# Clustered attention and two expert layers: where the first head's operands come from, and in which order TensorE takes its first work

## The reference

```python
q_assign = argmax(einsum('bhsd,hcd->bhsc', q_n, c_n), -1)      # q: 2 x 8 heads x 768 x 64, 16 clusters per head
k_assign = argmax(einsum('bhsd,hcd->bhsc', k_n, c_n), -1)      # q_n, k_n, c_n: rows divided by their norms
mask = q_assign[..., :, None] == k_assign[..., None, :]
scores = where(mask, q @ k.T / sqrt(D), -1e9)
attn = softmax(scores) @ v                                     # x: 1536 tokens x 512
x = gate * (relu(x @ w1[e]) @ w2[e])                           # e: the best of 8 experts for each token
out = ((x @ w_a) * (x @ w_b)) @ w_out
```

## Time and profile before

| | us |
|---|---|
| median of 3 runs | 815.81 (815.75 to 816.17) |
| the profiled execution | 815.89 |
| its span, first to last instruction | 814.1 |
| PE busy | 804.4 |
| DVE busy | 455.1 |
| ACT busy | 361.0 |
| POOL busy | 365.8 |

### The profile page before, as it was taken

One profiled execution on the slowest core, in us unless ns is written; L12 is line 12 of the kernel. 1 busy time (PEld: TensorE's weight loads), 2 busy tenths in 40 slices (PEclk: granted clock), 3 DMA queues, 4 the chain that ended last, 5 costly groups with the idle time before them and its releaser, 6 DMA issues.

```text
span 814.1 us, 13192 instructions
## 1 busy us (share of the span) xinstructions
PE 804.4 (99%) x4414; PEld 677.7 (83%) x4415; DVE 455.1 (56%) x721; ACT 361.0 (44%) x742; POOL 365.8 (45%) x308
## 2 busy tenths in 40 slices
PE   8999999999999999999999999999999999999997
PEld 5899999999997688888888888888888888888886
DVE  6987987987997989998866004531212112121211
ACT  6877877877886344334343443111212111121112
POOL 6788988988982355455455634000311002010001
PEclk9999999999999999999999999999999999999999
DMA  6563363363243577788667304300101000010001
GB/s 182 135 184 95 102 185 93 101 185 94 63 120 92 169 236 241 245 253 249 200 205 233 95 35 108 113 0 14 38 3 53 1 14 13 1 52 0 1 1 52
DMA packets 48665, 86.62 MB, mean 106 GB/s; under 512 B 17856, under 2 KB 19904, under 8 KB 48624
## 3 DMA queue, kind: packets, MB, share of 16 engines
q1 hardware_dynamic: 41888, 69.36, 29.5%
q0 software_dynamic: 3856, 11.33, 4.8%
q10 hardware_dynamic: 2880, 5.39, 1.7%
HBM read 73.29 MB, written 11.30 MB: 104 GB/s over the span
## 4 chain that ended last, share of the span: by engine, by line
PE 79%; issue 16%; DMA 2%; POOL 1%; DVE 1%; SPq 0%; POOLq 0%; ACT 0%; DVEq 0%; ACTq 0%
PE bank L1679 9%; PE bank L1749 9%; PE bank L1492 8%; PE bank L1646 7%; PE bank L1648 7%; PE bank L1647 7%; PE bank L1686 4%; PE bank L1461 4%; PE bank L1753 4%; PE bank L1482 4%; PE bank L1508 4%; PE bank L1510 3%; PE bank L1520 2%; PE bank L1419 2%; PE bank L1693 2%
## 5 line engine op out<-in xcount | busy, mean ns | idle before, releaser
L1383 DVE TENSOR_TENSOR ab_raw<-bank,a_sb 128x512 f32<-128x512 f32 x35 | 24.2, 691 | 187.7 <-PE bank L1648 187.7
L410 DVE CAST w_split<-stage 128x1024 fp32r<-128x1024 f32 x68 | 68.5, 1007 | 72.9 <-PE bank L1686 53.9
L1133 DVE TENSOR_REDUCE neg_max<-bank 128x1 f32<-128x768 f32 x96 | 91.2, 951 | 28.7 <-PE bank L1482 28.2
L414 DVE TENSOR_TENSOR w_split<-stage,w_split 128x1024 fp32r<-128x1024 f32 x72 | 98.3, 1369 | 2.4
L1101 DVE TENSOR_TENSOR pT_lo<-bank,pT_hi 128x384 fp32r<-128x384 f32 x192 | 97.3, 547 | 2.7 <-ACT pT_hi L847 2.6
L847 ACT ACTIVATE pT_hi<-bank 128x384 fp32r<-128x384 f32 x192 | 84.2, 491 | 32.0 <-PE bank L1492 30.2
L867 ACT ACTIVATE probs<-bank,neg_max 128x768 f32<-128x768 f32 x96 | 87.0, 907 | 11.6 <-DVE neg_max L1133 11.6
L714 POOL TENSOR_TENSOR hT_lo<-hT_raw,hT_hi 128x512 fp32r<-128x512 f32 x38 | 54.9, 1446 | 79.1 <-ACT hT_raw L926 78.9
L1492 PE MATMUL bank<-ident,probs 128*128 128x128 f32 x576 | 79.8, 274 | 0.9 <-DVE pT_lo L1101 0.9
L986 ACT ACTIVATE a_sb<-bank 128x512 f32<-128x512 f32 x35 | 20.9, 597 | 134.9 <-PE bank L1648 134.9
L1749 PE MATMUL bank<-w_split,hT_hi 128*128 (+1 forms) x304 | 79.5, 403 | 0.0
(11 more groups left out here) (264 smaller groups left out, 1736.7 us busy)
## 6 DMA issues: line engine op xcount, KB each, us to landing
stage<-w SPq DMA_DIRECT2D x64, 512.0 KB, 4.5
q_raw<-qT SPq DMA_DIRECT2D x32, 192.0 KB, 3.7
k_raw<-kT SPq DMA_DIRECT2D x32, 192.0 KB, 3.9
sorted_y<-y_sb ACTq DMA_DIRECT2D x19, 257.0 KB, 5.0
q_pair<-qT SPq DMA_DIRECT2D x8, 384.0 KB, 4.3
v_raw<-v_keys SPq DMA_DIRECT2D x16, 192.0 KB, 3.7
stage<-w_a SPq DMA_DIRECT2D x6, 512.0 KB, 4.7
stage<-w_b SPq DMA_DIRECT2D x6, 512.0 KB, 4.5
```

The costliest lines, as they stand in the source:

```text
L414: eng.tensor_tensor(dst[:, 1], stage[:, i % STAGES], dst[:, 0].bitcast(F32), ALU.subtract).then_inc(s_cv, 1)
L1133: dve.tensor_reduce(neg_max[:, qt % 2:qt % 2 + 1], scores[qt % 2][:, 0:S], AX_X, ALU.max, negate=True).then_inc(s_max, 1)
```

## The change

It gives head 0 two transfers instead of four: only the upper halves of `k_raw` and `q_raw` are loaded, keys first. The lower halves of `q_hh`, `q_raw`, `k_hl` and `k_hm` of head 0 are made from `q_pair` and `k_pair`, whose lower partitions hold head 0. ScalarE makes its five pieces ahead of `back_w` instead of behind it; `k_hm`'s copy goes from ScalarE to VectorE, ahead of the first `first_assign`. GpSimd's first low part waits for a semaphore of its own (`s_kh0`), which the upper key half sets. `reload_pair(1)` waits besides for the readers of the first pair's data. On TensorE both high products of head 0 stand ahead of the turned one-hots, with one spin ahead of them and three behind instead of five ahead; the one-hot transposes of head 1 get two spins ahead of them, and the two behind the similarities go. The similarities of pair 1 are done in tiles 2 to 5 of head 0 instead of 1 to 4, VectorE's steps on them in tiles 0, 1 and 2 of head 1 instead of tile 5 of head 0 and tiles 0 and 1, the one-hot transposes of pair 1 in tile 3 instead of 2. In all pairs, the steps of `assign` come ahead of `scale_x` where a tile has both.

```diff
@@ reload_pair
                 sp.wait_ge(s_sims, pp)
+                if static(pp) and pp == 1:
+                    for done in (s_qs, s_khi, s_khm):
+                        sp.wait_ge(done, 1)
@@ sync, start
-            load_rows(sp, 0, 0)
+            for raw, src in ((k_raw, kT), (q_raw, qT)):
+                sp.dma_start(raw[D:P, 0, :], src[0:1].rearrange("g d s -> (g d) s")).then_inc(s_qk[0], 16)
@@ prepare
-                pool.wait_ge(s_qk[slot], 64 * (turn + 1))
+                pool.wait_ge(s_qk[slot], 64 * turn + (32, 64)[slot])
@@ first_lows
-                pool.wait_ge(s_khi, g + 1)
+                pool.wait_ge(*((s_kh0, 1) if g == 0 else (s_khi, g + 1)))
...
-                pool.wait_ge(s_qhh, g + 1)
+                if g >= 1:
+                    pool.wait_ge(s_qhh, g + 1)
@@ scalar, start
+            act.wait_ge(s_pair, 32)
+            act.activation(q_hh[0:D, 0], q_pair[0:D], ACT.Copy, scale=float(D) ** -0.5)
+            act.activation(q_raw[0:D, 0], q_pair[0:D], ACT.Copy, scale=float(D) ** -0.5).then_inc(s_qs, 1)
+            act.wait_ge(s_qk[0], 32)
+            act.activation(k_hl[D:P, 0], k_raw[D:P, 0], ACT.Copy).then_inc(s_kh0, 1)
+            act.activation(k_hl[0:D, 0], k_pair[0:D], ACT.Copy).then_inc(s_khi, 1)
+            act.activation(q_hh[D:P, 0], q_raw[D:P, 0], ACT.Copy, scale=float(D) ** -0.5).then_inc(s_qhh, 1)
             act.wait_ge(s_const, 1)
             for half in range(2):
                 rows = slice(half * D, half * D + D)
                 act.activation(back_w[rows, :, 0:D], ...).then_inc(s_bw, 1)
-            first_key_high(0)
-            act.activation(q_hh[:, 0], q_raw[:, 0], ACT.Copy, scale=float(D) ** -0.5).then_inc(s_qhh, 1)
-            act.wait_ge(s_qhh, 1)
-            act.activation(q_raw[0:D, 0], q_raw[0:D, 0], ACT.Copy, scale=float(D) ** -0.5).then_inc(s_qs, 1)
-            act.activation(k_hm[0:D, 0], k_raw[0:D, 0], ACT.Copy).then_inc(s_khm, 1)
@@ vector, head
-                steps = {(0, 5): (0,), (1, 0): (1, 2), (1, 1): (3, 4)} if first else {
+                steps = {(1, 0): (0,), (1, 1): (1, 2), (1, 2): (3, 4)} if first else {
...
+                    for step in steps.get((slot, qt), ()) if more else ():
+                        assign(pp + 1, step)
                     if before and qt % GT == 2:
                         scale_x(g - 1, pp - 1 + slot, 1 - slot, qt // GT)
-                    for step in steps.get((slot, qt), ()) if more else ():
-                        assign(pp + 1, step)
@@ vector, start
             dve.memset(first_pair[:, :, :], 0.0).then_inc(s_yps, 1)
+            dve.wait_ge(s_pair, 32)
+            dve.tensor_copy(k_hm[0:D, 0], k_pair[0:D, :]).then_inc(s_khm, 1)
@@ tensor, head
-                sim_tiles = {qt: range(3 * qt - 3, 3 * qt) for qt in range(1, 5)} if first else {0: range(6), 1: range(6, 12)}
+                sim_tiles = {qt: range(3 * qt - 6, 3 * qt - 3) for qt in range(2, 6)} if first else {0: range(6), 1: range(6, 12)}
...
                     if first and (slot, qt) == (0, 1):
+                        spin(2)
                         pe.wait_ge(s_asgn, 15)
                         first_hot_transposes(first_hot_T, 2, s_hotT)
                         spin(2)
                     if more and slot == 0 and qt in sim_tiles:
                         similarities(pp + 1, sim_tiles[qt])
-                    if first and (slot, qt) == (0, 1):
-                        spin(2)
...
-                    if more and slot == 1 and qt == (2 if first else 1):
+                    if more and slot == 1 and qt == (3 if first else 1):
                         hot_transposes(pp + 1)
@@ tensor, start
-            spin(5)
+            spin(1)
             score_high(0, 0, 0)
+            score_high(0, 0, 1)
+            spin(3)
             pe.wait_ge(s_asgn, 10)
             first_hot_transposes(first_hot_k, 2, s_hotK)
             first_hot_transposes(first_hot_q, 0, s_hotQ)
-            score_high(0, 0, 1)
```

More of the change, by code:

```diff
@@ L268, in attention_moe_gate @@
         s_khi = sem("k_high_done")
+        s_kh0 = sem("first_k_high_copy_for_low_done")
         s_khl = sem("k_low_done")
@@ L812, in _, with first_key_high @@
             act.activation(exp_spare[:, :], cen_n[:, 1:2], ACT.Exp, scale=0.0)
+            def first_key_high(g):
+                act.wait_ge(s_qk[g], 64)
+                act.activation(k_hl[:, g], k_raw[:, g], ACT.Copy).then_inc(s_khi, 1)
+            act.wait_ge(s_pair, 32)
[5 more added lines that the diff above has]
+            act.activation(q_hh[D:P, 0], q_raw[D:P, 0], ACT.Copy, scale=float(D) ** -0.5).then_inc(s_qhh, 1)
             act.wait_ge(s_const, 1)
@@ L816, in _ @@
                 act.activation(back_w[rows, :, 0:D], ident[rows, rows].unsqueeze(1).to_broadcast([D, G, D]), ACT.Copy).then_inc(s_bw, 1)
-            def first_key_high(g):
-                act.wait_ge(s_qk[g], 64)
-                act.activation(k_hl[:, g], k_raw[:, g], ACT.Copy).then_inc(s_khi, 1)
-            first_key_high(0)
-            act.activation(q_hh[:, 0], q_raw[:, 0], ACT.Copy, scale=float(D) ** -0.5).then_inc(s_qhh, 1)
-            act.wait_ge(s_qhh, 1)
-            act.activation(q_raw[0:D, 0], q_raw[0:D, 0], ACT.Copy, scale=float(D) ** -0.5).then_inc(s_qs, 1)
-            act.activation(k_hm[0:D, 0], k_raw[0:D, 0], ACT.Copy).then_inc(s_khm, 1)
             def lay_gate_weights():
```

## The result

The changed kernel takes 819.62 us (median of 5 runs, 819.53 to 819.82), the kernel before 815.81 beside it (815.59 to 816.17): a ratio of 1.0046, 95% interval 1.0032 to 1.0061. The forecast was 816.0 with a range to 816.9. The profiled execution took 819.72 us with a span of 817.9, against 814.1 before, so the two profiles show the difference: 3.8 us.

The account below looks back on a forecast made before the run. TensorE is never idle from 35 us, so only when it becomes full counts: `x_head` 0.15 us earlier, one-hot transposes 0.33 paid, +0.18; 815.89 + 0.18 - 0.08 = 816.0 us, range 815.1 to 816.9.

Parts of the forecast that it names:

- Assignment steps one tile later: First pair, VectorE: same instructions, all still ahead of head 1's tile 2 `x_head`, which comes at 34.73 us, 0.15 earlier.
- Landing and ScalarE: Start: upper halves land at 7.9 us (other bound 9.89), upper `k_hl` copy at 8.19, `back_w` covered with 1 us to spare.
- GpSimd: Start: head 0's first low part begins at 9.19 us, 0.16 after its input, and ends at 11.0.
- VectorE's copy: Start: one 64x768 copy to fp32r takes 0.75 us, between 0.4 and 1.0, hidden in 1.26 us of idle time.
- The one-hot transposes: TensorE, head 0's start: they begin at 12.99 us instead of 13.29, -0.30 us.
- Tile 2's product: TensorE, head 0: it waits for the first exponential and moves from 17.77 to 17.47 us.
- Similarities in tile 5: Head 0's tile 5: their 0.59 us is paid, so head 1's first product goes from 25.24 to 25.53 us.
- `x_head`: VectorE, head 1's tile 2: 34.88 - 0.30 + 0.15 = 34.73 us, 0.15 earlier; TensorE's next product waits for it.
- the rival of the whole gain: Line 1507 is held by the transposes, not `x_head`, so the early start passes whole: 815.5 us; chance 0.22.
- The one-hot transposes in tile 3: Head 1's tile 3, where TensorE is full: their 0.33 us is paid, -0.15 + 0.33 = +0.18 us.
- Nothing more is lost: Head 1's tile 3: the transposes' ScalarE reader stands behind an exponential ending about when they end, so no further cost.
- The slower side: TensorE's clock falls in a new idle gap near the start, 2.4 us more: 818.3 us; chance 0.04.

Follow-up runs that it names:

- `order_first_pair`: The changed kernel with the assignment steps ahead of `scale_x` in the first pair only, behind it in all others: 816.48 us, ratio 1.001.
- `start_only`: The kernel before with only the new transfers, the new start of ScalarE, GpSimd and VectorE, and TensorE's new order up to tile 1: 815.61 us, ratio 1.0.

## Why the prediction was wrong

**The step that failed.** "Assignment steps one tile later" priced the new order for the first pair alone ("all still stand ahead of the `x_head` of tile 2 in head 1"). The diff swaps `assign` and `scale_x` for all pairs, and the sum has no term for the other six in which a tile has both. The sentences "All that the diff touches lies before 37 us" and "From there on I take a shift to be carried unchanged to the end" then shut them out, and so did my description of the kernel, by which the change touches only the start and the first pair: a TensorE that is full in 213.00 of 213.00 us was read as one that nothing can reach. It was full by hardly any margin. In tile 2 of a middle pair `x_head` came 0.46 us later and TensorE 0.43, so 0.03 us was free; in tile 5 the product starts 0.06 us after the end of `x_head` in both kernels, so by this reading none was. The price was to be had from rows of before: a step takes 0.47 us from start to start (82.10 to 82.57, where VectorE's next instruction starts), `x_head` ends at 82.18 and 89.25, and the products start at 82.36 and 89.31. Two places of at most 0.47 in six pairs would have given up to 5.6 us; it was 3.4.

**The other steps**, counted from the first `sim_max` (9.80 before, 9.51 after) because the two executions start 0.29 us apart. The rows of the changed kernel that answer to the earlier trace rows, ACT and POOL first:

```profile
8.09 0.84 ACT L827 ACTIVATE k_hl<-k_raw 64x768 fp32r<-64x768 f32 x1
...
10.69 2.14 ACT L833 ACTIVATE back_w<-ident 64x1024 f32<-64x1024 f32 x2
13.26 0.98 ACT L890 ACTIVATE k_hm<-bank,mask_line 16x768 fp32r<-16x768 bf16 x1 [0.43 <-PE bank L1460]
```

```profile
9.09 1.81 POOL L649 TENSOR_TENSOR k_hl<-k_raw,k_hl 64x768 fp32r<-64x768 f32 x1 [3.80 <-ACT k_hl L827]
```

DVE and PE:

```profile
8.16 0.53 DVE L1213 CAST k_hm<-k_pair 64x768 fp32r<-64x768 f32 x1
...
9.51 0.26 DVE L1229 TENSOR_REDUCE sim_max<-bank 128x6 f32<-128x96 f32 x1 [0.81 <-PE bank L1428]
...
34.49 0.37 DVE L1127 TENSOR_TENSOR x_head<-bank,row_inv 128x216 f32<-128x216 f32 x1
```

```profile
12.65 0.84 PE L1460 MATMUL bank<-ident_bf,one_hot 128*128 128x128 bf16 x12
...
14.39 0.93 PE L1491 MATMUL bank<-k_hm,q_lm 80*128 80x512 f32 x4 [0.89 <-POOL k_hm L661]
...
17.14 0.62 PE L1470 MATMUL bank<-k_hl,q_hh 128*128 128x512 f32 x2 [0.60 <-ACT probs L874]
...
25.28 0.60 PE L1470 MATMUL bank<-k_hl,q_hh 128*128 128x512 f32 x2
...
33.20 0.92 PE L1501 MATMUL bank<-ident,probs 128*128 128x128 f32 x6
35.01 0.41 PE L1516 MATMUL bank<-pT_hi,v_split 128*128 128x384 f32 x1 [0.89 <-DVE x_head L1127]
...
36.45 0.59 PE L1470 MATMUL bank<-k_hl,q_hh 128*128 128x512 f32 x2
```

- *Landing and ScalarE*: the upper key half was there for the copy at 8.09 us (forecast 8.19), and `back_w` ended ahead of the mask rows, which still waited 0.43 us for TensorE.
- *GpSimd*: 9.09, forecast 9.19.
- *VectorE's copy*: 0.53 us, forecast 0.75 between 0.4 and 1.0; hidden, 0.81 us of idle time are left behind it. The 1007 ns that I took for the nearest row are the mean of unlike durations: the middle one of these 68 casts takes 687 ns, the longest 1787. By columns, 687 ns gives 0.52 us.
- *The one-hot transposes*: 3.49 to 3.14 us behind `sim_max`, -0.35; forecast -0.30. Tile 2's product -0.34. A part of this is luck: against the other executions with the old start the same transposes gain between nothing and 0.28 us, as said above.
- *Similarities in tile 5*: head 1's first product goes from 15.44 to 15.77 us behind `sim_max`, +0.33; forecast +0.29.
- *`x_head`*: 25.08 to 24.98, -0.10; forecast -0.15. That `x_head` and not the transposes holds the product is now open to see: the transposes start at 33.20, and the 0.89 us behind them is a wait for `x_head`. This settles the rival of the whole gain, for the transposes are not what holds the product in this kernel.
- *The one-hot transposes in tile 3*: the high product behind them goes from 26.72 to 26.94, +0.22; forecast +0.18. "Nothing more is lost" was wrong by 0.10: the next high product follows after 2.49 us (36.45 to 38.94) and followed after 2.39 (36.52 to 38.91). At 43.56 us `order_first_pair` is 0.34 late where 0.18 was forecast; with the 0.25 of the stall in the last pair that makes 0.4 of the 0.5 us by which it lies above my 816.0.

**The rivals.** The slower side was named as a fall of TensorE's clock. The granted clock reads 1.00 in every window above, but it does so from 2 to 7 us too, where the first eleven spins take 4.30 us, so the distances decide. Behind idle stretches of 0.89 and 0.60 us the products keep theirs: from the high to the low product it is 0.45 us (17.14 to 17.59), as before (17.77 to 18.22). That is the higher of its two levels. The Trainium skill, "TensorE: Matmul & The Clock Gate", Part 1, has throttled as the default state that activity releases; here no idle stretch behind the start, up to the 0.89 us, was followed by a fall. The true slower side, one mechanism with its place and price, was in the diff, in a line that I had described as "in all pairs", and was not among the rivals.

## What to carry to other kernels

An edit in a loop body is priced in every iteration that runs it, above all where two instructions only change places: nothing is added, yet what is released second is released later by the time that the first one takes from start to start, 0.46 us here. That an engine is busy all the time doesn't say that nothing can make it late; what protects it is the lead of those that feed it: for each moved instruction, look up how long before its reader's start its result is there. And an order that a trace shows as a wait of 0.2 us may cost 0.4, or show no wait at all; measure between starts.

## What the runs showed besides

- The new start leaves no gain that can be measured: `start_only` is at 815.61 us against 815.65. What it wins against an execution with a late landing is 0.3 us, against one with an early landing nothing, and 0.25 us is lost again in the last pair. A margin that is read off one execution is worth no more than the spread between executions, 9.46 to 9.91 us for this landing.
- A copy of 64x768 to fp32r took 0.53 us on VectorE and 0.84 us on ScalarE. The mean of a group (1007 ns for the casts of the forecast) can lie far from its middle member (687 ns), so look at the spread before a row is used as a price.
